# Unit three's norm and the embedding's Newton step on GpSimd, with ScalarE's and TensorE's head in another order

## What is computed

```python
mag = np.sqrt(a_re * a_re + a_im * a_im)
scale = np.minimum(mag, 0.999) / (mag + 1e-06)
a_re_n, a_im_n = (a_re * scale, a_im * scale)
for t in range(S):
    new_re = ar * S_re - ai * S_im
    new_im = ar * S_im + ai * S_re
    S_re, S_im = (new_re + kv, new_im)          # kv is the outer product of k[t] and v[t]
    y[:, :, t] = np.einsum('bhd,bhde->bhe', q[:, :, t], S_re)
# first layer, on the 3072 rows of y
h = np.maximum(np.maximum(x @ w1, x @ w2), x @ w3)
x = h @ w_out
# second layer: one of 8 experts for each row
en = expert_emb / (np.linalg.norm(expert_emb, axis=-1, keepdims=True) + 1e-06)
logits = xn @ en.T / tau
expert_idx = np.argmax(logits, axis=1)
# out[row] = gate * (relu(x @ w1[e]) @ w2[e])
```

## Time and profile before

| what | value |
| --- | --- |
| median of 3 runs | 899.06 us (897.47 to 899.07) |
| the profiled execution | 897.5 us, with a span of 895.8 us |
| TensorE busy in the span | 797.3 us |
| VectorE, ScalarE, GpSimd busy | 648.2, 497.3 and 479.4 us |
| mean granted TensorE clock | 0.964 |

### The profile page before, as it was taken

How to read it: one execution, slowest core, us unless ns; L and a number is a source line. 1 busy time by engine, 2 the same in 40 slices (tenths; PEclk the granted TensorE clock), 3 DMA queues, 4 the chain that set the end, 5 groups by cost and what they waited for, 6 DMA issues and landing times.

```text
span 895.8 us, 18723 instructions
## 1 busy us (share of the span) xinstructions
PE 797.3 (89%) x6641; PEld 739.5 (83%) x6642; DVE 648.2 (72%) x1046; ACT 497.3 (56%) x1033; POOL 479.4 (54%) x768
## 2 busy tenths in 40 slices
PE   0568898799899999999999999949999999999995
PEld 0446797689789898988999999938999999997894
DVE  5989899799999999999897755287323353558721
ACT  5696966676868777787666563234211242437511
POOL 1199999899979797979765000013223233334222
PEclk9769999989999999999999999958999999999998
DMA  9501152352424242432421110444511142417211
GB/s 303 137 9 45 49 148 83 95 153 77 119 76 112 76 130 83 116 85 70 96 69 42 42 51 21 151 167 171 192 35 59 48 165 67 167 49 282 85 36 45
DMA packets 41875, 89.73 MB, mean 100 GB/s; under 512 B 6264, under 2 KB 23680, under 8 KB 40480
## 3 DMA queue, kind: packets, MB, share of 16 engines
q1 hardware_dynamic: 37632, 76.04, 27.7%
q0 software_dynamic: 4160, 12.60, 4.3%
HBM read 69.74 MB, written 17.69 MB: 98 GB/s over the span
## 4 chain that ended last, share of the span: by engine, by line
PE 54%; DVE 20%; POOL 9%; issue 8%; ACT 5%; DMA 2%; ACTq 0%; DVEq 0%; SPq 0%; POOLq 0%
PE yu L1795 4%; PE yu L1796 4%; PE yu L1799 4%; PE mm L1795 4%; PE mm L1796 4%; PE mm L1799 4%; POOL c_re L2165 2%; POOL c_im L2173 2%; POOL ring L2176 2%; PE tr L2067 2%; PE mm L2067 2%; PE mm L2069 2%; PE tr L2069 2%; PE tr L2068 2%; PE mm L2068 2%
## 5 line engine op out<-in xcount | busy, mean ns | idle before, releaser
L1795 PE MATMUL mm<-up_hi,x_hi 128*128 128x384 f32 x432 | 157.0, 363 | 12.3 <-DVE h_sb L1239 8.8
L2165 POOL TENSOR_TENSOR c_re<-ring 112x128 f32<-112x128 f32 x165 | 125.5, 761 | 51.1 <-DVE ring L1192 37.6
L1796 PE MATMUL mm<-up_lo,x_hi 128*128 128x384 f32 x432 | 147.1, 341 | 0.0
L2250 POOL DMA_INDIRECT out_rows<-g_o,rows_out x30 | 35.3, 1175 | 145.3 <-DVE g_o L1647 136.7
L1795 PEld LDWEIGHTS mm<-up_hi,x_hi 128*128 128x128 f32 x432 | 82.1, 190 | 21.3 <-DVE h_sb L1239 11.9
L1799 PE MATMUL mm<-up_hi,x_lo 128*128 128x384 f32 x432 | 99.2, 338 | 0.0
L2169 POOL TENSOR_TENSOR c_im<-turn,ring 112x128 f32<-112x128 f32 x105 | 74.4, 708 | 28.9 <-ACT turn L735 28.7
L2226 POOL DMA_INDIRECT g_in<-x_scratch,rows_in x34 | 37.2, 1095 | 94.5 <-DVE rows_in L1610 69.2
L1796 PEld LDWEIGHTS mm<-up_lo,x_hi 128*128 128x128 f32 x432 | 82.4, 191 | 0.0
L1795 PE MATMUL yu<-e_hi,gh_hi 128*128 128x384 f32 x240 | 82.2, 342 | 0.0
L1796 PE MATMUL yu<-e_lo,gh_hi 128*128 128x384 f32 x240 | 80.7, 336 | 0.0
(11 more groups left out here) (264 smaller groups left out, 2352.2 us busy)
## 6 DMA issues: line engine op xcount, KB each, us to landing
raw<-in_moe_w SPq DMA_DIRECT2D x16, 1536.0 KB, 9.1
a_dn<-in_a_laid SPq DMA_DIRECT2D x18, 384.0 KB, 6.2
an_scratch<-a_dn SPq DMA_DIRECT2D x18, 384.0 KB, 2.3
ring<-an_scratch SPq DMA_DIRECT2D x18, 384.0 KB, 5.5
q_in<-in_q_laid SPq DMA_DIRECT2D x24, 224.0 KB, 2.8
k_in<-in_k_laid SPq DMA_DIRECT2D x24, 224.0 KB, 3.4
v_in<-in_v_laid SPq DMA_DIRECT2D x24, 192.0 KB, 3.4
x_scratch<-x_sb SPq DMA_DIRECT2D x24, 192.0 KB, 3.2
```

The lines of the kernel that those rows point to most:

```text
L1795: nc.tensor.matmul(out, hi[:, x, :], w_hi(x), start=(x == 0), stop=False)
L1796: nc.tensor.matmul(out, hi[:, x, :], w_lo(x), start=False, stop=False)
L2165: nc.gpsimd.tensor_tensor(c_re[:, 0:count, :, :], cur, bc(prev[:, :, 0, :], 2, 2), ALU.mult).then_inc(chain_prod, 1)
```

## The change

Three things are changed, all ahead of the loop over chunks. VectorE's queue loses the norm of unit 3 but for one operation (`norm_scale`), `norm_m2` of unit 2 and the embedding's operations up to its reciprocal. GpSimd's queue gets them, ahead of group 1's product, in forms with one more instruction for each that took two steps in one. ScalarE's and TensorE's heads are written in another order, and so is the end of VectorE's: `norm_m2(4)` now stands behind all seven joins, and `norm_m2(5)` and `norm_sum(5)` behind `k_decay(0)`.

```diff
@@ ScalarE
             norm_square(2, norm_of(2))
             split_up(0)
             norm_mag(2, norm_of(2))
+            norm_square(3, norm_of(3))
...
             emb_columns()
-            norm_square(3, norm_of(3))
-            router_rows(0)
             norm_rsqrt(2, norm_of(2))
             norm_mag(3, norm_of(3))
+            router_rows(0)
+            low_copy(range(0, 2))
+            norm_rest(2, norm_of(2))
+            norm_rsqrt(3, norm_of(3))
             split_up(1)
-            norm_rsqrt(3, norm_of(3))
-            norm_rest(2, norm_of(2))
+            router_cols(0)
             router_rows(1)
             norm_rest(3, norm_of(3))
+            low_copy(range(2, 6))
+            router_cols(1)
+            router_rows(2)
             norm_square(4, norm_of(4))
-            router_cols(0)
-            router_rows(2)
-            router_cols(1)
+            low_copy(range(6, 8))
+            router_cols(2)
             split_up(2)
-            router_cols(2)
-            low_copy(range(0, 4))
-            split_dn()
-            low_copy(range(4, 8))
-            norm_square(5, norm_of(5))
+            low_copy(range(8, 10))
             norm_mag(4, norm_of(4))
             stage_z(0)
             z_square(0)
+            low_copy(range(10, 12))
+            norm_square(5, norm_of(5))
+            z_recip(0)
+            split_dn()
             norm_mag(5, norm_of(5))
-            z_recip(0)
-            low_copy(range(8, 12))
@@ VectorE
+            def norm_scale(m, s):
+
+                dve.wait_ge(rest_ready, m + 1)
+                nc.vector.scalar_tensor_tensor(s.m2, s.la, MAXMAG, s.rr, ALU.mult, ALU.min).then_inc(scale_ready, 1)
...
-            norm_m2(2, norm_of(2))
             first_chain(1)
+            norm_sum(2, norm_of(2))
             first_chain(2)
-            norm_m2(3, norm_of(3))
-            norm_sum(2, norm_of(2))
             first_chain(3)
+            norm_inverse(2, norm_of(2))
             first_chain(4)
-            norm_sum(3, norm_of(3))
-            norm_inverse(2, norm_of(2))
             first_chain(5)
+            norm_apply(2, norm_of(2))
             first_chain(6)
-            norm_inverse(3, norm_of(3))
-            norm_apply(2, norm_of(2))
+            norm_scale(3, norm_of(3))
             first_chain(7)
-            norm_apply(3, norm_of(3))
-            for number in range(4):
+            for number in range(7):
                 join(0, number)
             norm_m2(4, norm_of(4))
-            for number in range(4, 7):
-                join(0, number)
-            norm_m2(5, norm_of(5))
+            z_norm(0)
             norm_sum(4, norm_of(4))
-            z_norm(0)
-            norm_sum(5, norm_of(5))
             z_newton(0)
             q_decay(0)
             k_decay(0)
+            norm_m2(5, norm_of(5))
+            norm_sum(5, norm_of(5))
@@ TensorE
             router(0)
-            router(1)
             low_parts(range(0, 2))
             router_product(0)
+            low_parts(range(2, 4))
+            router(1)
+            low_parts(range(4, 6))
+            router_product(1)
             router(2)
-            low_parts(range(2, 4))
-            router_product(1)
+            low_parts(range(6, 8))
             router_product(2)
-            low_parts(range(4, 12))
+            low_parts(range(8, 12))
@@ GpSimd
+            def norm_sum(m, s):
+                pool.wait_ge(sum_ready, m)
+                pool.wait_ge(mag_ready, m + 1)
+                nc.gpsimd.tensor_scalar(s.la, s.la, EPS * EPS, None, ALU.add).then_inc(norm_part, 1)
+                pool.wait_ge(norm_part, 3)
+                nc.gpsimd.tensor_tensor(s.m2, s.la, s.m2, ALU.add).then_inc(sum_ready, 1)
...
+            emb_max()
+            emb_newton()
+            norm_m2(2, norm_of(2))
+            norm_m2(3, norm_of(3))
+            norm_sum(3, norm_of(3))
+            norm_inverse(3, norm_of(3))
+            norm_apply(3, norm_of(3))
             chain_steps(1, range(1, 11))
```

More of the change, by code:

```diff
@@ L299, in attention_moe_program @@
         emb_tr = sem("emb_tr")
+        norm_part = sem("norm_part")
         emb_ready = sem("emb_ready")
@@ L1184, in norm_inverse, with norm_apply @@
                 nc.vector.scalar_tensor_tensor(s.la, s.rr, 1.5, s.la, ALU.add, ALU.mult).then_inc(inverse_ready, 1)
-            def norm_apply(m, s):
+            def norm_scale(m, s):
                 dve.wait_ge(rest_ready, m + 1)
                 nc.vector.scalar_tensor_tensor(s.m2, s.la, MAXMAG, s.rr, ALU.mult, ALU.min).then_inc(scale_ready, 1)
+            def norm_apply(m, s):
+                norm_scale(m, s)
                 dve.wait_ge(scale_ready, m + 1)
@@ L1306, in _ @@
             norm_m2(0, norm_of(0))
-            emb_max()
             norm_sum(0, norm_of(0))
             norm_m2(1, norm_of(1))
-            emb_square()
-            emb_half()
-            emb_newton()
             first_square(0, norm_of(0))
@@ L1317, in _ @@
             norm_apply(0, norm_of(0))
-            emb_norm()
-            emb_eps()
             emb_inverse()
@@ L1743, in emb_columns @@
                 pe.wait_ge(s_const, 1)
-                pe.wait_ge(emb_step, 11)
+                pe.wait_ge(emb_step, 13)
                 for x in range(KX):
@@ L2192, in turns, with emb_max, emb_newton @@
                 nc.gpsimd.tensor_tensor(r[:, :, 1, :], rp[:, 0, :, 1, :], rp[:, 1, :, 0, :], ALU.add).then_inc(rot_ready, 1)
+            def emb_max():
+                pool.wait_ge(emb_step, 1)
+                nc.gpsimd.tensor_scalar(emb_s[:, 1:2], emb_s[:, 0:1], TINY, None, ALU.max).then_inc(emb_step, 1)
+            def emb_newton():
+                pool.wait_ge(emb_step, 4)
+                nc.gpsimd.tensor_tensor(emb_s[:, 4:5], emb_s[:, 3:4], emb_s[:, 3:4], ALU.mult).then_inc(emb_step, 1)
+                pool.wait_ge(emb_step, 5)
+                nc.gpsimd.tensor_tensor(emb_s[:, 5:6], emb_s[:, 1:2], emb_s[:, 4:5], ALU.mult).then_inc(emb_step, 1)
+                pool.wait_ge(emb_step, 6)
+                nc.gpsimd.tensor_scalar(emb_s[:, 6:7], emb_s[:, 5:6], -0.5, 1.5, ALU.mult, ALU.add).then_inc(emb_step, 1)
+                pool.wait_ge(emb_step, 7)
+                nc.gpsimd.tensor_tensor(emb_s[:, 7:8], emb_s[:, 6:7], emb_s[:, 3:4], ALU.mult).then_inc(emb_step, 1)
+                pool.wait_ge(emb_step, 8)
+                nc.gpsimd.tensor_tensor(emb_s[:, 4:5], emb_s[:, 1:2], emb_s[:, 7:8], ALU.mult).then_inc(emb_step, 1)
+                pool.wait_ge(emb_step, 9)
+                nc.gpsimd.tensor_scalar(emb_s[:, 5:6], emb_s[:, 4:5], EPS, None, ALU.add).then_inc(emb_step, 1)
+                pool.wait_ge(emb_step, 10)
+                nc.gpsimd.tensor_tensor(emb_s[:, 6:7], emb_s[:, 5:6], tau_sb[:, 0:1], ALU.mult).then_inc(emb_step, 1)
@@ new lines, in norm_m2 @@
+            def norm_m2(m, s):
+                pool.wait_ge(asq_ready, m + 1)
+                pool.wait_ge(a_normed, m - 1)
+                re, im = planes(s.a_sq)
+                nc.gpsimd.tensor_scalar(s.m2, re, TINY, None, ALU.max).then_inc(norm_part, 1)
+                pool.wait_ge(norm_part, 1 if m == 2 else 2)
+                nc.gpsimd.tensor_tensor(s.m2, s.m2, im, ALU.add).then_inc(m2_ready, 1)
+            def norm_sum(m, s):
[4 more added lines that the diff above has]
+                nc.gpsimd.tensor_tensor(s.m2, s.la, s.m2, ALU.add).then_inc(sum_ready, 1)
@@ new lines, in norm_inverse @@
+            def norm_inverse(m, s):
+                pool.wait_ge(inverse_ready, m)
+                pool.wait_ge(rr_ready, m + 1)
+                nc.gpsimd.tensor_tensor(s.rr, s.m2, s.rr, ALU.mult).then_inc(norm_part, 1)
+                pool.wait_ge(norm_part, 4)
+                nc.gpsimd.tensor_scalar(s.rr, s.rr, -0.5, 1.5, ALU.mult, ALU.add).then_inc(newton_ready, 1)
+                pool.wait_ge(newton_ready, m + 1)
+                nc.gpsimd.tensor_tensor(s.la, s.rr, s.la, ALU.mult).then_inc(inverse_ready, 1)
@@ L2194, in _, with norm_apply @@
+            def norm_apply(m, s):
+                pool.wait_ge(a_normed, m)
+                pool.wait_ge(scale_ready, m + 1)
+                nc.gpsimd.tensor_tensor(s.a_in, s.a_in, bc(s.m2, len(list(s.m2.shape)) - 1, 2), ALU.mult).then_inc(a_normed, 1)
+            emb_max()
[5 more added lines that the diff above has]
+            norm_apply(3, norm_of(3))
             chain_steps(1, range(1, 11))
```

27 lines of the change are left out of this document (3 added, 24 removed).

## The result

The changed kernel takes 908.68 us (median of 4 runs, 906.77 to 909.08), the kernel before in the same comparison 898.26 (897.30 to 899.07). The ratio is 1.0113, with a 95% interval of 1.0096 to 1.0131: 10.2 us slower, 8.6 to 11.8 (all differences in time here are worked out from such a ratio; the two medians lie 10.4 apart). Forecast were 4.5. The profiled execution took 909.08 us, at the upper end of its runs, so its span is 11.6 above the one before.

The account below looks back on a forecast made before the run. VectorE's queue up to `norm_apply(5)`, for which GpSimd's group 2 waits, was taken to set the pace. Terms -0.8 (T) and +5.3 gave +4.5 us, 902.0 on the profiled execution, 903.6 as forecast time; whole range 899.5 to 907.5.

Parts of the forecast that it names:

- Up to J: Stage to the end of group 0's joins: 52.1 us plus 1.0 for engines hindering each other, 53.1 against 55.65 before.
- J: End of group 0's last join on VectorE; forecast at 53.1 us, lower bound 50.7.
- unit 3's ring: Unit 3's norm passing through ScalarE and GpSimd, ending with norm_rest(3) at 36.7 us; VectorE waits some 1.4 for it.
- The upper bound of +3: Most that hindrance adds up to J: ring's GpSimd operations take 45% more, +2.3, and +3 with ScalarE's operations caught later.
- The prices on GpSimd: Wide operations on GpSimd at 2.2 ns an element: two inputs 1.3 us for 512, 2.4 for 1024; one input 0.65.
- From J to T: From the joins' end to chunk 0's z_newton(0) (T): 8.31 us instead of 6.56, giving T = 61.4.
- From T to `norm_apply(4)`: From z_newton(0) to norm_apply(4): 13.2 us instead of 7.92, 5.3 more, as norm_m2(5) comes only behind k_decay(0).
- G2: Start of GpSimd's first link of group 2, 83.13 us before; forecast at 87 to 88.
- The engines exclude each other: Rival, chance 0.12: VectorE waits for whole wide GpSimd operations, three waits, about 4 us more; +8.5, 907.6.
- Less lost: Rival, chance 0.10: J at its lower bound of 50.7, so +2.1 in all, 901.
- given back later: Rival, chance 0.10: gaps between 125 and 170 us or on TensorE give back most of the 4.5; 899 to 900.
- faster: Rival, chance 0.06: GpSimd leaves VectorE's joins alone and they run as fast as links; -2.1, 897.

Follow-up runs that it names:

- e7: Changed kernel with each wide two-input operation on GpSimd cut into pieces of 128 elements; 908.15 us, ratio 1.0120 to the kernel before.
- e2: Kernel before with only the new order of the end of VectorE's and ScalarE's heads, all norms on VectorE; 903.42 us, ratio 1.0066.
- e5: Kernel before with only unit 5's norm late, norm_m2(4) left between the joins; 903.46 us, ratio 1.0071.
- e1: Changed kernel with the end of VectorE's and ScalarE's heads in the old order, unit 3 still on GpSimd; 900.79 us, ratio 1.0032 to the kernel before.
- e3: Changed kernel with unit 3's norm and norm_m2(2) back on VectorE; 905.22 us, ratio 1.0080 to the kernel before.
- e6: Kernel before with only norm_m2(4) behind all seven joins, unit 5's norm early as before; 900.08 us, ratio 1.0021.
- e9: Kernel before plus five unused two-input operations of 512 elements on idle GpSimd beside the first links; 901.31 us, ratio 1.0040.
- e10: Kernel before plus five unused one-input operations of 512 elements on idle GpSimd beside the first links; 899.11 us, ratio 1.0012.

## Why the prediction was wrong in size

**The failed step is "Up to J": the hindrance taken as +1.0.** It put J at 53.1, and J was 58.7. The mechanism was wrong there and not only the size: the forecast has VectorE wait 1.4 us for unit 3's ring, and the trace has it held, one operation after the other. VectorE's own queue would have had it at 50.7, as worked out there. Onto that came no wait at `norm_scale(3)` (it started at 40.89 without idle time), but stretches: 7.6 us behind the first link, and 0.7 by which that link itself came later than the 23.5 computed. That is 59.0, against 58.7. The upper bound of +3 was no bound, since it was worked out from the wrong row: joins take 45% more than links, so I let GpSimd's operations grow by 45%. What grows is VectorE's, and not in proportion to anything of its own: it grows by what is left of GpSimd's operation. The row that had it was the 1.44 us beside 1.36, the other way round: there VectorE's product began first and GpSimd's operation ended 0.3 us after it. And of the joins it could be seen that widths of 64 and 128 elements hold for no more than 0.3 to 0.5 us, because that is all that such an operation lasts.

**The ring was mis-sized too**, which the missing wait hides. `norm_rest(3)` on ScalarE ended at 40.58, where 36.7 were forecast, and only 0.3 ahead of VectorE's arrival:

```profile
39.86 0.72 ACT L721 ACTIVATE n_rr<-n_la,one_col 112x512 f32<-112x512 f32 x1 [1.10 <-POOL n_la L2206]
```

`norm_rsqrt(2)` started at 26.56 instead of 25.5, `norm_sum(3)` on GpSimd lasted 3.05 us instead of 2.05, `norm_inverse(3)` 4.71 instead of 3.4. From 40.58, with 0.6 for the scale, 1.3 for link 7 and 13.4 for the joins, J would be 55.9 with nothing held behind it, and 54.8 without the 1.1 us by which `norm_rsqrt(2)` was late. That is an estimate from these rows; by it, taking the holding away would not have brought back all of the 5.6 us.

**The prices on GpSimd.** Two inputs of 512 were put at 1.3 us and measured 1.28 to 1.58 (2.12 for one beside VectorE's product and a link), the product of 1024 at 2.4 and measured 2.41: right in the main. One input was put at half, 0.65, and measured 1.14 to 2.31; it is 0.62 where VectorE is idle (`e7`, at 41.00). The Trainium skill, GPSIMD Engine Reference, section "3.1 Elementwise — side-by-side cycle accounting", has 4,497 ns for an addition of 2048 elements, which is 2.2 ns an element. The trace agrees: from 1.28 us for 512 to 2.41 for 1024 it is 2.2 ns for each further element.

**From J to T:** 8.31 forecast, counted from the start of VectorE's next operation; counted so, 8.11 measured (8.03 from the last join's end, and 8.03 in `e2` too). Right.

**From T to `norm_apply(4)`:** 13.2 forecast, 13.98 measured. Right in mechanism, as `e5` shows alone; the 0.7 on top is that VectorE's operations between `z_newton(0)` and `norm_m2(5)` took 5.40 us instead of 4.68, beside GpSimd's links. ScalarE's idle time was 4.22 instead of "some 3" for the same reason.

**Behind it:** VectorE's way from there to group 2 was 1.2 us shorter than before. GpSimd's wait ahead of group 2 was 14.7 us, where "some 6" were forecast: besides the 9.4 by which group 2 is late, GpSimd took 33.7 us for group 1 (44.21 to 77.88) instead of 39.7 (42.24 to 81.96). VectorE was busy for 24.27 of 34 us beside it, against 35.75 of 41; that this is why is argued, not shown. It gained nothing, since GpSimd only waits longer. From G2 on, 9.4 late, nothing was given back: in the profiled execution the chunks' `x_hi` between 285 and 565 us come 10.7 to 11.0 later than before, and the time is 10.2 later. So the consequence drawn from the earlier trace rows, that GpSimd's start of group 2 sets the pace, held. Over the runs the time follows it: +2.8 there and +2.9 in time for `e1`, +5.3 and +5.9 for `e2`, +6.6 and +7.2 for `e3`, +1.5 and +1.9 for `e6`, +5.3 and +6.4 for `e5`, +3.0 and +3.6 for `e9`. `e10` is the exception, with +2.7 there and +1.1 in time, whose interval reaches to +2.6. In its profiled execution `x_hi` comes 1.7 to 2.0 later between 285 and 565 us, and the span is 1.0 longer, so there a part was given back; where and why stays open.

**The sum.** Forecast was -2.55 (J) + 1.75 + 5.3 = +4.5. Measured was +3.0 + 1.5 + 6.1 - 1.2 = +9.4 at group 2, and 10.2 at the end. Of the 5.7 that were missing, 5.6 are J's; the others (-0.2, +0.8, -1.2 and the 0.8 behind group 2's start) nearly cancel. Between the two profiled executions, 11.6 apart, it is 2.2 behind group 2's start. No experiment was made for these. TensorE stood for 20.66 us until `z_newton(0)` (6.57 before) and 7.22 ahead of its outer product (1.86 before), which then took 1.94 us instead of 1.13, at a granted clock of 0.81 from 82 to 100 us (1.00 before); chunk 0's `x_hi` came 11.5 us late instead of 9.4, and VectorE's `x_lo` waited 1.92 for it, as the last line of its timeline shows. That is where I would look, and it is argued, not shown.

**The rivals.** "The engines exclude each other" was the right mechanism at half its size: three waits of 1.2 to 1.4 us were priced, and there were six, one of them of 2.2. Its 907.6 lies 1.1 below the measured time, and I had left it out of the range because of its small chance, though the wide operations were to be counted in the change itself: six with two inputs, each beside a VectorE queue that was never idle. "Less lost", "given back later" and "faster" fell: J went the other way, nothing came back, and VectorE was not left alone.

## What to carry to other kernels

Work that is moved from a full VectorE to GpSimd is paid for twice if it has two inputs: charge VectorE with nearly the whole of GpSimd's duration (here 1.0 to 1.1 us for each operation of 512 elements, which took 0.7 on VectorE itself), and look for a place where VectorE is idle. Cutting it in pieces frees VectorE and makes GpSimd slow instead, so it should help only where nobody waits for GpSimd; no run here tests that. And where two queues pass a norm back and forth, an operation that is put behind a long block on one is late by that block on the other, with all that is queued there: unit 5's two short operations, set back by 4.7 us, cost 6.4.

## What was not expected of the hardware

- An operation on GpSimd with two inputs held a VectorE operation that began after it till it ended: links' operations of 0.42 us took 1.15 to 1.50 and 2.59, one of 0.29 took 1.36, and a one-input operation (`TENSOR_SCALAR`, 20.83) took 1.37 instead of 0.43. GpSimd's own duration for 512 elements was 1.28 to 1.58 us after the change, but for the one that began beside VectorE's product (37.71), which took 2.12. One VectorE operation was held for each of GpSimd's.
- In the cases seen, the one that began second was held: VectorE's in the six of the change, GpSimd's in the row of before, where it began 0.24 us after VectorE's product and took 1.44 us instead of 0.46.
- With one input it is nearly the other way round: VectorE's operations grew by 0.3 to 0.4 us, GpSimd's from 0.62 to between 1.1 and 2.3.
- Four operations of 128 elements on GpSimd took 2.3 to 3.4 us beside a busy VectorE, and 1.7 beside an idle one (`e7`, at 39.20 and 41.70); the same 512 elements in one took 1.3 to 1.6.
